# Splitting the row sums' reciprocals over 128 partitions by way of DRAM, one addition of exponentials moved to GpSimd, and the copies of an attention stage put in another order

## The chip, the cores and the metric

One core of one Trainium2 chip. The metric is the device time of one execution in microseconds. The core's engines, which run their own instruction streams and meet at semaphores: TensorE (PE), VectorE (DVE), ScalarE (ACT), GpSimd (POOL), and SyncE (SP), which here issues nearly all DMA transfers, in the order in which they are written.

## The reference

```python
# attention: batch 2, 8 heads, 768 tokens, head size 64
q_bits = (q @ proj > 0); k_bits = (k @ proj > 0)          # 6 sign bits each
mask = bucket(q_bits) == bucket(k_bits)                   # keys of the same bucket only
scores = where(mask, q @ k.T / 8, -1e9)
attn = exp(scores - max(scores)); attn /= (sum(attn) + 1e-9)
x = attn @ v                                              # to (1536 tokens, 512)
# layer 1
h = x @ w_in1 ; x = (maximum(h, 0) + alpha * minimum(h, 0)) @ w_out1      # 512 -> 2048 -> 512
# layer 2
h = x @ w_in2
P = a0 + a1*h + a2*h^2 + a3*h^3 ; Q = 1 + |b0|*|h| + |b1|*h^2
out = (P / (Q + 1e-6)) @ w_out2
```

All is float32. The kernel splits operands into a high part (fp32r) and the rest, and multiplies high by high, high by low and low by high.

## The kernel before, in words

**Attention** goes over 16 heads in 8 pairs; pair `j` holds heads `h = 2j + u`, u = 0 or 1, and u is also the slot of double-buffered tiles. Pairs 1 to 5 are one hardware loop (`over_pairs`), pairs 0, 6 and 7 are written out. `left` is 2 in all pairs but the last two (1, 0). A head has six chunks of 128 keys. For each chunk TensorE makes scores (keys on partitions, 768 queries in two halves; `scores_one` L534 and `scores_two` L539, two chunks ahead), ScalarE takes the exponential into `p[c]` (L696), and TensorE multiplies it with v (`values`, L560) into `ps_o`. Chunks go in groups of two (`begin` = 0, 2, 4); in a group come the scores, the first list of helper steps, in group 0 the two steps below, the values, then the second list.

Ahead of their head, for one or two heads later, run: **bits** (L475), sign bits of q and k, turned by VectorE (L984) into `bit01` and by GpSimd (`bit_rows`, L831) into the penalty rows `pen`; **a** (L479), the plain scores with penalty, of which VectorE takes row maxima from PSUM (L980, halves of 384; `s_a_free` counts them); and **m** (`turn`, L490/492), which transposes maxima and empty-row marks that GpSimd made (`row_stats`, `v_partial`). ScalarE copies these out (`stat_rows`, L743/745) and SP carries the stats into `q2` (`fill_stats`, L419); VectorE makes `v_sum` (L1004) from them.

In group 0, ahead of the values, stand `empty_rows` (L573), which starts the accumulation in `ps_o` for rows without a key, and `sums` of the head before (L584): 24 small matmuls with ones over `p_sum[0..2]`. VectorE makes each `p_sum[n] = p[2n] + p[2n+1]` (`add`, L1013), one behind each group. ScalarE copies the sums, 768 queries as 4 rows of 192 spread over 128 partitions in copies, to `den_row[u]` (L757); VectorE takes reciprocals of all 128x192 (L124), SP stores 4 rows to DRAM (`store_rows`, L112) and, once per pair, spreads them over 64 partitions each (`spread`, L120). GpSimd multiplies (`normalise`, L908), ScalarE and GpSimd split the result into `x_hi` and `x_lo`.

**The order is written out by hand** in each engine's `pair`. SP's, per head h: stats of head h+1, raw q and k of head h+4, v, the reciprocals' store of head h-1, then `fill_a` for head h+3 (high parts L355/356, penalty rows L360/361), `spread` (u = 0), and the eight copies into the operands of head h+2 (`fill_b_hi` L374 to L377, waits for the last values of head h; `fill_b_lo` L381 to L384). The high part itself is ScalarE's `split_qk` (L678), behind the exponential of step c = 4; it waits for the last copies that read this slot (`s_a_in`, `s_b_in`). GpSimd's `split_qk` (L822) makes the low part.

**The MLP layers** (from L1101) run over 3 tiles of 512 tokens and 16 chunks of 128 hidden columns. Weights of four chunks are split beforehand, the others during layer 1: SP loads them (`load`, L1206/1209), GpSimd splits (L1241 to L1252). The first two `up` chunks run inside the last pair.

Of the kernel before, what the change touches and what calls it, by code (L numbers as in the profile page):

```python
# [62 lines left out]
def build_program(nc, qk, v, proj, w_in1, w_out1, alpha, w_in2, w_out2, a, b, consts, out):  # L63
    rden_dram = nc.dram_tensor("rden_scratch", (PAIRS, 2, S), F32, kind="Internal").ap()
    outer = ExitStack()
    with outer:
# [23 lines left out]
        x32, rden_bc = work[:, 0:S], work[:, S:2 * S]  # L90
        guard = sb_in(outer, "guard", [P, 1])

        s_sums = sem("s_sums")
        s_rden = [sem(f"s_rden{u}") for u in range(2)]
        s_rst = [sem(f"s_rst{u}") for u in range(2)]
# [12 lines left out]
        def store_rows(sp, u, j, row):  # L108

            sp.wait_ge(s_rden[u], j + 1)  # L110
            dst = rden_dram[bass.ds(j, 1)].rearrange("a u (n t) -> (a u n) t", n=4)[4 * u:4 * u + 4]
            sp.dma_start(dst, row[0:P:QUARTER_ROWS]).then_inc(s_rst[u], 16)  # L112
# [19 lines left out]
        with att:  # L132
# [90 lines left out]
            s_add = sem("s_add")  # L223
            s_summed = sem("s_summed")
            s_pv = sem("s_pv")
            s_head = sem("s_head")
# [113 lines left out]
            def attention_sync(sp):  # L340
# [22 lines left out]
                def fill_a(u, jj):  # L363
                    g = 2 * jj + u
                    fill_a_hi(u, g)
                    fill_a_pen(u, g)

                def fill_b_hi(u, jj):
# [3 lines left out]
                    if due(g - 1):  # L372
                        sp.wait_ge(s_head, g - 1)
# [37 lines left out]
                def fill_stats(slot, jj):  # L411
# [3 lines left out]
                    if due(g - 1):  # L415
                        sp.wait_ge(s_head, g - 1)
# [17 lines left out]
                def pair(j, left):  # L434
                    for u in range(2):
                        h = 2 * j + u
                        if left == 1 and u == 0:
# [7 lines left out]
                        if isinstance(j, int) and j == 0:  # L445
# [15 lines left out]

            def attention_tensor(pe):
# [91 lines left out]
                def values(slot, h, c, t):  # L554

                    pe.wait_ge(s_exp, t + 1)
                    if c == 0:
                        pe.wait_ge(s_vhi, h + 1)
                    for i in range(2):
                        m = pe.matmul(ps_o[OUT[i], 0, 0:HALF], v_use[slot][:, c], p[c][:, i * HALF:(i + 1) * HALF],  # L560
                                      start=False, stop=(c == KC - 1))
                    m.then_inc(s_head if c == KC - 1 else s_pv, 1)

                def empty_rows(slot, h):

                    if isinstance(h, int) and h == 0:
                        pe.wait_ge(s_first_sum, 1)
                    else:
                        pe.wait_ge(s_a_free, turned(h))
                    if due(h):  # L570
                        pe.wait_ge(s_evac, h)
                    for i in range(2):
                        pe.matmul(ps_o[:, 0, 0:HALF], v_sum[slot][:, (1 - i) * D:(1 - i) * D + P],  # L573
# [1061 lines left out]
```

## Time and profile before

| | us |
|---|---|
| median of 3 runs | 853.35 |
| lowest, highest | 848.66, 853.62 |
| the profiled execution | 848.33 |
| its span in the profile | 846.3 |
| mean granted clock of TensorE | 0.969 of full |

| engine | busy us | share |
|---|---|---|
| TensorE, matmuls | 802.2 | 95% |
| VectorE | 558.6 | 66% |
| ScalarE | 358.3 | 42% |
| GpSimd | 269.7 | 32% |

Attention ends near 315 us, with the last sums' matmuls. An engine that waits shows as idle, and the profile names the engine or transfer that released it. The granted clock is a share of TensorE's full clock (2.4 GHz; the other level is 1.2). A share of busy time is a mean over stages with different limits, so the views by stretch of time say more than the totals.

### The profile page before, as it was taken

How to read it: one execution, taken by the hardware profiler on the slowest of the kernel's cores; microseconds unless marked ns; L12 is line 12 of the kernel's file. 1: busy time of each engine (PE TensorE's matmuls, PEld its weight loads, DVE VectorE, ACT ScalarE, POOL GpSimd, SP SyncE). 2: the span in 40 equal slices, each digit the busy share in tenths (PEclk: the TensorE clock that was granted, in tenths of full speed). 3: DMA queues.
4: the chain of work that ended last, by engine and by line, in shares of the span. 5: the costliest groups of instructions: out<-in, count | busy, mean ns of one | idle time of the engine just before them, and what ended most of it. 6: DMA issues, size and time to landing. Idle time of an engine off the chain costs nothing.

```text
span 846.3 us, 11668 instructions
## 1 busy us (share of the span) xinstructions
PE 802.2 (95%) x3820; PEld 589.4 (70%) x3820; DVE 558.6 (66%) x830; ACT 358.3 (42%) x588; POOL 269.7 (32%) x341
## 2 busy tenths in 40 slices
PE   8898888888888999999999999999999999999998
PEld 5455545454444667888888888888788888888886
DVE  6776676666666746544434344338988888888886
ACT  7343444434333541111201121116766676667664
POOL 7563443535355345970000017777000000000000
PEclk9999999988888999999999999999999999999999
DMA  4564464545444623420000003332000010001001
GB/s 127 146 179 130 111 156 110 129 112 135 119 131 119 149 72 117 119 81 1 0 1 1 13 0 100 92 95 75 1 2 1 0 50 2 0 1 50 2 1 50
DMA packets 29726, 58.75 MB, mean 69 GB/s; under 512 B 5420, under 2 KB 9300, under 8 KB 29684
## 3 DMA queue, kind: packets, MB, share of 16 engines
q1 hardware_dynamic: 29396, 58.16, 25.4%
q8 instruction: 25, 0.41, 0.2%
q14 instruction: 17, 0.14, 0.1%
q10 hardware_dynamic: 288, 0.04, 0.0%
HBM read 29.54 MB, written 3.19 MB: 39 GB/s over the span
## 4 chain that ended last, share of the span: by engine, by line
PE 82%; DVE 7%; DMA 4%; SPq 4%; issue 2%; ACT 0%; POOL 0%; DVEq 0%; ACTq 0%
PE acc L1311 29%; PE ps_h L1279 29%; PE ps_o L560 6%; PE ps_a L479 4%; DMA ka<-pen 3%; PE ps_s L534 3%; PE ps_s L539 3%; PE ps_o L584 3%; PE ps_a L475 2%; DVE den_row L124 2%; PE ps_o L573 1%; DVE row_max L980 1%; SPq L360 1%; SPq L112 1%; SPq L356 1%
## 5 line engine op out<-in xcount | busy, mean ns | idle before, releaser
L1344 ACT ACTIVATE g_hi<-num 128x512 fp32r<-128x512 f32 x96 | 59.9, 624 | 207.4 <-PE acc L1311 203.0
L1414 DVE TENSOR_TENSOR g_lo<-num,g_hi 128x512 fp32r<-128x512 f32 x96 | 70.7, 736 | 78.4 <-ACT g_hi L1344 77.9
L696 ACT ACTIVATE p<-ps_s 128x768 f32<-128x768 f32 x96 | 77.5, 810 | 98.1 <-PE ps_s L539 98.1
L980 DVE TENSOR_REDUCE row_max<-ps_a 128x1 f32<-128x384 f32 x180 | 90.9, 546 | 35.4 <-PE ps_a L479 33.6
L479 PE MATMUL ps_a<-ka,qa 76*128 76x384 f32 x180 | 63.3, 408 | 33.4 <-DMA ka<-pen 31.4
L1013 DVE TENSOR_TENSOR p_sum<-p 128x768 f32<-128x768 f32 x48 | 68.6, 1431 | 27.7 <-PE ps_o L584 27.2
L479 PEld LDWEIGHTS ps_a<-ka,qa 76*128 76x128 f32 x180 | 31.9, 196 | 68.9 <-issue 36.4
L1279 PE MATMUL ps_h<-x_hi,w_late_in_hi 128*128 128x512 f32 x288 | 78.9, 395 | 1.0 <-POOL w_late_in_lo L1243 1.0
L1279 PE MATMUL ps_h<-x_hi,w_late_in_lo 128*128 128x512 f32 x288 | 77.7, 392 | 0.0
L1279 PE MATMUL ps_h<-x_lo,w_late_in_hi 128*128 128x512 f32 x288 | 77.6, 391 | 0.0
L560 PE MATMUL ps_o<-p,v_use 128*64 128x384 f32 x384 | 73.7, 502 | 0.0
L1422 DVE TENSOR_SCALAR num<-ps_h,alpha_sb 128x512 f32<-128x512 f32 x48 | 36.0, 750 | 55.9 <-PE ps_h L1279 53.3
L1352 ACT ACTIVATE den_q<-ps_h,abs_b 128x512 f32<-128x512 f32 x48 | 33.1, 690 | 82.7 <-PE ps_h L1279 76.5
L1279 PEld LDWEIGHTS ps_h<-x_hi,w_late_in_hi 128*128 128x128 f32 x288 | 54.0, 188 | 13.8 <-POOL w_late_in_lo L1243 1.4
L1279 PEld LDWEIGHTS ps_h<-x_lo,w_late_in_hi 128*128 128x128 f32 x288 | 54.1, 188 | 12.1
L1279 PEld LDWEIGHTS ps_h<-x_hi,w_late_in_lo 128*128 128x128 f32 x288 | 54.1, 188 | 12.0
L1311 PE MATMUL acc<-w_late_out_hi,g_hi 128*128 128x512 f32 x144 | 56.8, 395 | 0.0
L1311 PE MATMUL acc<-g_hi,w_late_out_hi 128*128 128x512 f32 x144 | 56.6, 393 | 0.0
L1311 PE MATMUL acc<-w_late_out_lo,g_hi 128*128 128x512 f32 x144 | 56.5, 392 | 0.0
L1311 PE MATMUL acc<-g_hi,w_late_out_lo 128*128 128x512 f32 x144 | 56.5, 392 | 0.0
L1311 PE MATMUL acc<-g_lo,w_late_out_hi 128*128 128x512 f32 x144 | 56.2, 390 | 0.0
L1311 PE MATMUL acc<-w_late_out_hi,g_lo 128*128 128x512 f32 x144 | 56.1, 390 | 0.0
(167 smaller groups left out, 1584.0 us busy)
## 6 DMA issues: line engine op xcount, KB each, us to landing
stage<-in_w_in SPq DMA_DIRECT2D x26, 256.0 KB, 2.8
stage<-in_w_out SPq DMA_DIRECT2D x26, 256.0 KB, 2.8
raw<-in_qk SPq DMA_DIRECT2D x15, 384.0 KB, 3.2
q<-hi SPq DMA_DIRECT2D x30, 192.0 KB
k<-hi SPq DMA_DIRECT2D x30, 192.0 KB
v_raw<-in_v SPq DMA_DIRECT2D x16, 192.0 KB, 3.0
work<-rden_scratch SPq DMA_DIRECT2D x16, 192.0 KB, 3.4
out<-y SPq DMA_DIRECT2D x12, 256.0 KB, 2.5
```

Source lines behind the costliest of these rows:

```text
L479: m = pe.matmul(ps_a[:, i, 0:HALF], qa[slot][0:BIT_ROW + 12, c * P:(c + 1) * P], ka[slot][0:BIT_ROW + 12, half], start=True, stop=True)
L534: pe.matmul(ps_s[c % 2][:, i, 0:HALF], k1[slot][:, c * P:(c + 1) * P], q1[slot][:, i * HALF:(i + 1) * HALF], start=True, stop=False)
L560: m = pe.matmul(ps_o[OUT[i], 0, 0:HALF], v_use[slot][:, c], p[c][:, i * HALF:(i + 1) * HALF], start=False, stop=(c == KC - 1))
L696: nc.scalar.activation(halves(p[c][:]), ps_s[c % 2][:, :, 0:HALF], ACT.Exp, scale=float(D) ** -0.5).then_inc(s_exp, 1)
L980: dve.tensor_reduce(row_max[slot][:, i, c:c + 1], ps_a[:, i, 0:HALF], AX.X, ALU.max).then_inc(s_a_free, 1)
L1013: dve.tensor_tensor(p_sum[n][:], p[2 * n][:], p[2 * n + 1][:], ALU.add).then_inc(s_add, 1)
L1279: m = pe.matmul(ps_h[f % 4][:], weight(w, f)[:, k * P:(k + 1) * P], tile_cols(x, t, k), start=(n == 0), stop=(n == 3 * DK - 1))
L1311: m = pe.matmul(acc[d][:], lhs, rhs, start=(f == 0 and n == 0), stop=(f == FC - 1 and n == 2))
L1344: nc.scalar.activation(g_hi[f % 2][:], num[f % 4][:], ACT.Copy).then_inc(s_ghi, 1)
L1352: nc.scalar.activation(den_q[f % 2][:], h, ACT.Abs, scale=abs_b[:, 0:1])
L1414: dve.tensor_tensor(g_lo[f % 2][:], num[f % 4][:], g_hi[f % 2][:], ALU.subtract).then_inc(s_glo, 1)
L1422: dve.tensor_scalar(num[f % 4][:], h, 0.0, alpha_sb[:, f:f + 1], ALU.min, ALU.mult).then_inc(s_step, 1)
```

## The change

The order of heads, chunks and helper steps on TensorE stays; `empty_rows` goes from ahead of the values to behind those of chunk 3, so the values of chunk 0 start the accumulation. `p_sum[1]` (chunks 2 and 3) is made by GpSimd. The copied sums go to DRAM as they are; per pair, they are read back as 6 values per partition and slot, VectorE takes the reciprocals of 128x12 values once, behind the last group of the even head, and they go to DRAM again ahead of `spread`. ScalarE's `split_qk` goes from step 4 to step 1. SP's order is new, and the b copies wait for `empty_rows` and no longer for the last values.

```diff
+        def store_sums(sp, u, j, h, row):
+            sp.wait_ge(s_sums, h + 1)
+            dst = den_dram[bass.ds(j, 1)].rearrange("a u (n t) -> (a u n) t", n=4)[4 * u:4 * u + 4]
+            sp.dma_start(dst, row[0:P:QUARTER_ROWS]).then_inc(s_dst[u], 16)
+        def turn_sums(sp, j):
+            for u in range(2):
+                sp.wait_ge(s_dst[u], 16 * (j + 1))
+            if due(j):
+                sp.wait_ge(s_rden, j)
+            for u in (1, 0):
+                src = den_dram[bass.ds(j, 1)].rearrange("a u s -> (a u) s")[u:u + 1].rearrange("a (p c) -> (a p) c", c=KC)
+                sp.dma_start(den[:, u], src).then_inc(s_den, 16)
+        def store_rows(sp, j):
+            sp.wait_ge(s_rden, j + 1)
+            dst = rden_dram[bass.ds(j, 1)].rearrange("a u (p c) -> p (a u) c", c=KC)
+            sp.dma_start(dst, rden[:]).then_inc(s_rst, 16)
         def spread(sp, j):
+            sp.wait_ge(s_rst, 16 * (j + 1))
             for u in range(2):
-                sp.wait_ge(s_rst[u], 16 * (j + 1))
-            for u in (1, 0):
...
-        def reciprocal(dve, u, h, row):
-            dve.wait_ge(s_sums, h + 1)
-            dve.reciprocal(row, row).then_inc(s_rden[u], 1)
+        def reciprocals(dve, j):
+            dve.wait_ge(s_den, 32 * (j + 1))
+            if due(j):
+                dve.wait_ge(s_rst, 16 * j)
+            dve.reciprocal(rden[:], den[:]).then_inc(s_rden, 1)
...  SP, fill_b_hi and fill_stats
-                        sp.wait_ge(s_head, g - 1)
+                        sp.wait_ge(s_rows, g - 1)
...  SP, pair(j, left), for u in range(2)
-                        if left or u == 0:
-                            fill_stats(1 - u, j + u)
                         if left > 1:
                             load_raw(u, j + 2)
                         if left:
                             load_v(u, j + 1)
...
-                        if not (isinstance(h, int) and h == 0):
-                            store_rows(sp, 1 - u, j - 1 + u, den_row[1 - u][:])
+                        if first and u == 0:
+                            fill_stats(1 - u, j + u)
                         if left > 1 or (left == 1 and u == 0):
-                            fill_a(1 - u, j + 1 + u)
-                        if u == 0 and not (isinstance(j, int) and j == 0):
-                            spread(sp, j - 1)
+                            fill_a_hi(1 - u, h + 3)
+                        if not (first and u == 0):
+                            store_sums(sp, 1 - u, j - 1 + u, h - 1, den_row[1 - u][:])
+                        if (left or u == 0) and not (first and u == 0):
+                            fill_stats(1 - u, j + u)
+                        if left > 1 or (left == 1 and u == 0):
+                            fill_a_pen(1 - u, h + 3)
+                        if u == 0 and not first:
+                            turn_sums(sp, j - 1)
                         if left:
                             fill_b_hi(u, j + 1)
+                        if u == 0 and not first:
+                            store_rows(sp, j - 1)
                         if left:
                             fill_b_lo(u, j + 1)
+                        if u == 0 and not first:
+                            spread(sp, j - 1)
...  TensorE, values(slot, h, c, t), c == 0
+                        if due(h):
+                            pe.wait_ge(s_evac, h)
...
-                                      start=False, stop=(c == KC - 1))
-                    m.then_inc(s_head if c == KC - 1 else s_pv, 1)
+                                      start=(c == 0), stop=(c == KC - 1))
+                    m.then_inc(s_pv, 1)
...  TensorE, sums(h)
-                    pe.wait_ge(s_add, KC // 2 * (h + 1))
+                    pe.wait_ge(s_add, 2 * (h + 1))
+                    pe.wait_ge(s_add_too, h + 1)
...  TensorE, pair
-                            if begin == 0:
-                                empty_rows(u, h)
-                                if not first:
-                                    sums(h - 1)
+                            if begin == 0 and not first:
+                                sums(h - 1)
                             for c in range(begin, begin + group):
                                 values(u, h, c, KC * h + c)
+                                if c == 3:
+                                    empty_rows(u, h)
...  ScalarE, exponential(c, h, t)
-                        act.wait_ge(s_add, KC // 2 * (h - 1) + c // 2 + 1)
...
+                        if c // 2 == 1:
+                            act.wait_ge(s_add_too, h)
                         else:
-                            act.wait_ge(s_pv, (KC - 1) * (h - 1) + c + 1)
+                            act.wait_ge(s_add, 2 * (h - 1) + c // 4 + 1)
+                        act.wait_ge(s_pv, KC * (h - 1) + c + 1)
...  ScalarE, pair
+                            if c == (4 if first and u == 0 else 1) and (left > 1 or (left == 1 and u == 0)):
+                                split_qk(1 - u, j + 1 + u)
                             if c == 3 and not last:
                                 copy_v(1 - u, j + u)
-                            if c == 4 and (left > 1 or (left == 1 and u == 0)):
-                                split_qk(1 - u, j + 1 + u)
-                            if c == (2 if final else 3) and u == 1 and not first:
+                            if c == (2 if final else 5) and u == 1 and not first:
                                 x_high(act, j - 1)
...  GpSimd
+                def add(n, h):
+                    pool.wait_ge(s_exp, KC * h + 2 * n + 2)
+                    if due(h):
+                        pool.wait_ge(s_summed, h)
+                    nc.gpsimd.tensor_tensor(p_sum[n][:], p[2 * n][:], p[2 * n + 1][:], ALU.add).then_inc(s_add_too, 1)
...  GpSimd, pair: normalise from ahead of bit_rows to behind split_qk
                         if left > 1 or (left == 1 and u == 0):
                             bit_rows(1 - u, j + 1 + u)
+                        add(1, h)
+                        if left > 1 or (left == 1 and u == 0):
+                            split_qk(1 - u, j + 1 + u)
...  VectorE, pair
-                                if side == 0 and (begin + group) % 2 == 0:
+                                if side == 0 and begin + group in (2, KC):
                                     add((begin + group) // 2 - 1, h)
-                            if begin == 2 and not (first and u == 0):
-                                reciprocal(dve, 1 - u, h - 1, den_row[1 - u][:])
+                            if begin == 4 and u == 0 and not first:
+                                reciprocals(dve, j - 1)
...  handover to the MLP, SP
-                store_rows(sp, 1, PAIRS - 1, rden_bc[:, 0:QUARTER])
+                store_sums(sp, 1, PAIRS - 1, HEADS - 1, rden_bc[:, 0:QUARTER])
+                turn_sums(sp, PAIRS - 1)
+                store_rows(sp, PAIRS - 1)
                 spread(sp, PAIRS - 1)
```

## Rows read from the trace of the kernel before

**Rows 1.** The page, TensorE's granted clock in 40 equal slices, tenths of full.
```profile
PEclk9999999988888999999999999999999999999999
```
**Rows 2.** Stretches: busy time (instructions) per engine, granted clock, DMA share, GB/s.
```profile
160.00:200.00 40.00, 34.38 (x184) 19.95 (x182) 26.11 (x40) 15.65 (x26) 16.57 (x26) 0.83 0.49 124
...
280.00:320.00 40.00, 39.98 (x255) 26.08 (x255) 24.48 (x34) 20.97 (x36) 17.17 (x24) 1.00 0.39 101
```
**Rows 3.** TensorE's waits, whole span: total us, times, longest.
```profile
PE ps_a L479 <- DMA ka<-pen: 31.4, 12, 2.9
...
PE ps_h L1279 <- POOL w_late_in_lo L1243: 1.0, 1, 1.0
```
**Rows 4.** The chain of waits, 165 to 174 us: start, us, what.
```profile
166.41 1.27 DVE den_row L124
...
167.83 0.61 SPq L112
...
170.65 2.29 DMA ka<-pen
```
**Rows 5.** TensorE's timeline, marks of several heads: start, us, engine, line, operation.
```profile
39.73 0.52 PE L534 MATMUL ps_s<-q,k 128*128 128x384 f32 x2
...
41.91 0.84 PE L475 MATMUL ps_a<-raw,pj 128*24 128x384 f32 x4
42.69 0.62 PE L573 MATMUL ps_o<-q,v_sum 128*128 128x384 f32 x2
...
47.05 0.51 PE L479 MATMUL ps_a<-ka,qa 76*128 76x384 f32 x2
...
156.29 1.01 PE L573 MATMUL ps_o<-q,v_sum 128*128 128x384 f32 x2
...
169.44 0.52 PE L534 MATMUL ps_s<-q,k 128*128 128x384 f32 x2
...
173.06 1.00 PE L479 MATMUL ps_a<-ka,qa 76*128 76x384 f32 x2 [2.74 <-DMA ka<-pen]
...
258.49 1.01 PE L573 MATMUL ps_o<-q,v_sum 128*128 128x384 f32 x2
...
276.77 0.51 PE L573 MATMUL ps_o<-q,v_sum 128*128 128x384 f32 x2
...
290.23 0.51 PE L573 MATMUL ps_o<-q,v_sum 128*128 128x384 f32 x2
```
**Rows 6.** The stretch behind the wait of head 8, columns as rows 2.
```profile
174.00:179.30 5.30, 5.30 (x35) 2.45 (x33) 2.02 (x4) 0.81 (x1) 0.00 (x0) 0.53 0.76 182
```
**Rows 7.** VectorE, ScalarE, GpSimd near head 8; first, L1013's min/median/max in ns.
```profile
L1013 DVE TENSOR_TENSOR p_sum<-p x48: 894/964/2396, 24.4 to 311.5; 128x768 f32<-128x768 f32 x48
...
161.45 0.29 DVE L1004 SCALAR_TENSOR_TENSOR v_sum<-vs_hi,cst,ps_a 4x64 fp32r<-4x64 f32 x1 [1.32 <-ACT vs_hi L745]
...
167.16 0.84 ACT L678 ACTIVATE hi<-raw 128x768 fp32r<-128x768 f32 x1
...
168.08 1.83 POOL L822 TENSOR_TENSOR lo<-raw,hi 128x768 fp32r<-128x768 f32 x1 [1.12 <-ACT hi L678]
...
168.46 2.26 DVE L1013 TENSOR_TENSOR p_sum<-p 128x768 f32<-128x768 f32 x1
...
171.68 0.17 DVE L994 TENSOR_REDUCE top<-row_max 128x6 f32<-128x12 f32 x1
```
**Rows 8.** DMA issues: queue, count, KB each, median us to landing.
```profile
ab_raw<-in_b SPq DMA_DIRECT2D x1, 1.0 KB, 3.3
```
**Rows 9.** SP's issues in head 8, first and last of the four b-lo copies.
```profile
174.02 0.73 SPq L381 DMA_DIRECT2D k<-lo  x1
...
176.74 0.77 SPq L384 DMA_DIRECT2D k<-pen  x1
```
**Rows 10.** The handover to the MLP: VectorE's last reciprocal, SP's next load of weights.
```profile
323.15 1.35 DVE L124 RECIPROCAL work<-work 128x192 f32<-128x192 f32 x1
...
327.45 0.57 SPq L1206 DMA_DIRECT2D stage<-in_w_in  x1
```

More of the change, by code:

```diff
@@ L90, in build_program @@
         x32, rden_bc = work[:, 0:S], work[:, S:2 * S]
+        den = sb_in(outer, "den", [P, 2, KC])
+        rden = sb_in(outer, "rden", [P, 2, KC])
         guard = sb_in(outer, "guard", [P, 1])
         s_sums = sem("s_sums")
-        s_rden = [sem(f"s_rden{u}") for u in range(2)]
-        s_rst = [sem(f"s_rst{u}") for u in range(2)]
+        s_dst = [sem(f"s_dst{u}") for u in range(2)]
+        s_den = sem("s_den")
+        s_rden = sem("s_rden")
+        s_rst = sem("s_rst")
         s_rbc = sem("s_rbc")
@@ L223, in build_program @@
             s_add = sem("s_add")
+            s_add_too = sem("s_add_too")
             s_summed = sem("s_summed")
             s_pv = sem("s_pv")
-            s_head = sem("s_head")
+            s_rows = sem("s_rows")
             s_evac = sem("s_evac")
@@ L436, in pair @@
                         h = 2 * j + u
+                        first = isinstance(j, int) and j == 0
                         if left == 1 and u == 0:
                             stage_early(2)
-                        if left or u == 0:
-                            fill_stats(1 - u, j + u)
                         if left > 1:
@@ L444, in pair @@
                             load_v(u, j + 1)
-                        if isinstance(j, int) and j == 0:
+                        if first:
                             stage_early(u)
@@ L558, in values @@
                         pe.wait_ge(s_vhi, h + 1)
+                        if isinstance(h, int) and h == 0:
+                            pe.wait_ge(s_first_sum, 1)
+                        if due(h):
+                            pe.wait_ge(s_evac, h)
                     for i in range(2):
                         m = pe.matmul(ps_o[OUT[i], 0, 0:HALF], v_use[slot][:, c], p[c][:, i * HALF:(i + 1) * HALF],
-                                      start=False, stop=(c == KC - 1))
-                    m.then_inc(s_head if c == KC - 1 else s_pv, 1)
+                                      start=(c == 0), stop=(c == KC - 1))
+                    m.then_inc(s_pv, 1)
                 def empty_rows(slot, h):
-                    if isinstance(h, int) and h == 0:
-                        pe.wait_ge(s_first_sum, 1)
-                    else:
+                    if not (isinstance(h, int) and h == 0):
                         pe.wait_ge(s_a_free, turned(h))
-                    if due(h):
-                        pe.wait_ge(s_evac, h)
                     for i in range(2):
-                        pe.matmul(ps_o[:, 0, 0:HALF], v_sum[slot][:, (1 - i) * D:(1 - i) * D + P],
-                                  q2[slot][:, i * HALF:(i + 1) * HALF], start=(i == 0), stop=False)
+                        m = pe.matmul(ps_o[:, 0, 0:HALF], v_sum[slot][:, (1 - i) * D:(1 - i) * D + P],
+                                      q2[slot][:, i * HALF:(i + 1) * HALF], start=False, stop=False)
+                    m.then_inc(s_rows, 1)
                 def sums(h):
-                    pe.wait_ge(s_add, KC // 2 * (h + 1))
+                    pe.wait_ge(s_add, 2 * (h + 1))
+                    pe.wait_ge(s_add_too, h + 1)
                     if due(h):
@@ L940, in pair @@
                             row_stats(1 - u, h + 1)
-                        if u == 1 and not final and not (isinstance(j, int) and j == 0):
-                            normalise(j - 1)
                         if left > 1 or (left == 1 and u == 0):
                             bit_rows(1 - u, j + 1 + u)
+                        add(1, h)
+                        if left > 1 or (left == 1 and u == 0):
+                            split_qk(1 - u, j + 1 + u)
                         if left == 1 and u == 0:
@@ L947, in pair @@
                         if u == 1 and not final and not (isinstance(j, int) and j == 0):
+                            normalise(j - 1)
                             x_low(j - 1)
-                        if left > 1 or (left == 1 and u == 0):
-                            split_qk(1 - u, j + 1 + u)
                         if isinstance(j, int) and j == 0:
@@ L1529, in mlp_vector @@
                 step(0, 0, 0, False, None)
-                reciprocal(dve, 1, HEADS - 1, rden_bc[:, 0:QUARTER])
+                reciprocals(dve, PAIRS - 1)
                 def tile(layer, t, final):
```

23 lines of the change are left out of this document (7 added, 16 removed).

## The prediction

> **What bounds the kernel now.** The page comes first: TensorE's clock row sags in slices 9 to 14 and is full afterwards [rows 1]; a reader is to see a stage there that the rest of the span doesn't resemble. The view by stretches says where there is something to gain: from 160 to 200 us TensorE is busy 34.38 of 40 us at a mean clock of 0.83, from 280 to 320 us 39.98 of 40 at 1.00 [rows 2]. The two MLP layers behind are TensorE work without gaps, and the change doesn't touch them. So only attention, some 315 of 846 us, can move. Third, the waits of TensorE: 31.4 us in 12 waits, all for the same transfer, the penalty rows of `ka` [rows 3]. One per head, in heads 2 to 13.
>
> Fourth, the chain of waits through one of them, in head 8 [rows 4]. VectorE's reciprocal (1.27) ends, SP stores its rows (0.61), and behind that, in SP's order, stand the four copies into `qa` and `ka`; the last lands 2.29 us after its issue, and TensorE starts again at 173.06 after 2.74 us [rows 4, 5]. The wait costs twice: from 174.0 to 179.3 the granted clock is 0.53, near 1.2 of 2.4 GHz [rows 6]. In the timeline the empty-rows matmul, one pair per head, marks the heads: 42.69 in head 1, 276.77 in head 13, so 234.1 us for twelve heads, 19.5 each. From head 13 to head 14 TensorE doesn't wait: 13.46 us [rows 5].
>
> **What a head costs without the wait.** The head 13 stretch lacks two pieces, the bits matmuls (0.84, of which 0.8 in sequence) and one row-maximum pair (0.51 with its overlap, 0.4 in sequence) [rows 5]: 13.46 + 1.2 = 14.7; 14.8 with a little for VectorE's order. Twelve heads make 177.6.
>
> **The change, part by part.** *The penalty transfer.* ScalarE's split of q and k goes from behind chunk 4 to behind chunk 1; SP fills `qa`/`ka` before the sums' store, and no reciprocal stands in the way. I count from T, the start of the scores of chunk 2 (169.44 in head 8) [rows 5]. ScalarE copies the sums near T+4.2 (42.69 - 39.73 = T+3.0 in head 1, where the sums' matmuls begin, and some 1.2 us of them), splits by T+5.1, and SP issues two hi copies, the store (0.6), the stats, two penalty copies: done by T+9.4, landed (2.3) by T+11.7. It is wanted after T+15. All twelve old waits go: that is the 31.4 us and the low clock behind them.
>
> *The reciprocals.* Per head 1.34 us on 192 elements goes, for one of 12 elements per pair; the nearest row for a tiny operation is 0.17 [rows 7]. The pair's sums make a round trip: store, two loads of 24-byte pieces, reciprocal, store in 24-byte pieces, spread. No such transfer is in the trace; the nearest moves 1.0 KB in small pieces, 8 bytes to a partition, and lands in 3.3 us; the two steps of the store seen here are an issue of 0.61 and a landing near the 2.29 of the penalty rows [rows 4, 8]. I take 2.5, the nearer to the size, with both ends kept, and SP issues of 0.6. Loads are issued by T+10.9 in the even head and landed by T+13.4; VectorE asks for them only behind the last maximum of that head, 2.2 us into the next. Four microseconds of cover; past that it costs one for one.
>
> The Trainium skill (DMA: Bandwidth & Descriptors, "Why small descriptors are slow") holds small pieces to and from HBM to be slow, and speaks against this layout. The one small row at 3.3 us against 2.29 is no proof either way; by that rule the cover would shrink, and the sum would not change before it is used up.
>
> *What it leaves late.* SP's order in the even head is: turn, b-hi copies, wait for the reciprocals, store, b-lo copies. The reciprocals come 2.2 us into the odd head (its top reduction stands at 171.68, T+2.2, with a reciprocal less ahead of it) [rows 7]. Store to T+2.9; the four b-lo copies take 3.5 (174.02 to 177.51), to T+6.4 [rows 9]; landing 2.3, to T+8.7. ScalarE's split, now at chunk 1, waits for exactly these copies, and it arrives at T+4.2. Behind it in ScalarE's queue stand the stats copy and the partial-sum copy, and VectorE's `v_sum` behind them: 0.84 and 0.29 [rows 7], and some 0.3 at most for each small copy between, an estimate, to T+10.1. TensorE gets to the second half of the next row-maximum pair at 47.05 - 39.73 = 7.3 in head 1, 6.8 without the empty rows that move back [rows 5]. So it waits 3.3 us, in every odd head that has this split: 1, 3, 5, 7, 9, 11 (head 1 because SP is late from the weights). Six waits for twelve. The clock's fall after a wait cost from nothing to 2.9 us: from head 7 (156.29) to head 12 (258.49) a head takes 20.4 us, and 20.4 - 14.8 - 2.74 = 2.9; from head 1 to head 7 18.9, which leaves 1.4, and the reciprocals may account for it all [rows 5]. I take 1.5, since a pair has one wait where it had two. Odd heads: +4.8, six times, 28.8.
>
> *The even heads.* Copies to the odd head's operands end near T+21.7 of a 19.6 us head, landed at about T+2.1 of the next: no wait there. SP's own queue per pair is some 23 us of issues and 2 more, in 34.
>
> *The addition on GpSimd.* VectorE loses one of three additions (0.96 alone); GpSimd gains one that costs what its own of this shape costs, 1.83 [rows 7]. GpSimd is busy 16.57 of 40 us in 160 to 200 [rows 2], some 8.5 per head, and would be at 10.3 in 17. Its end matters to the sums matmuls and two exponentials of the next head, five us later. Cost nothing, the cover being those five us.
>
> *Empty rows behind chunk 3, the waits on counts:* same work, no cost; the b copies may start earlier, but SP isn't free earlier.
>
> *The handover to the MLP.* Before, the last store waits for a reciprocal that VectorE reaches at 323.15, and the late weights are issued at 327.45 [rows 10]. Now the store goes at about 318, loads landed by 323.3, reciprocal at 323.4, store, landing, spread, weights at 327.2. A wash; the 1.0 us wait of TensorE stays [rows 3].
>
> **The sum.** 177.6 + 28.8 = 206.4 for 234.1: minus 27.7 on the profiled execution of 848.3 (span 846.3), so 820.6. That execution is like the lowest of the three runs (848.66); their median is 5 us higher, where the same difference gives 825.7. I forecast 822. Bounds from the open terms: no odd waits at all, 791.8; odd waits with the full clock loss (37.2) and 1.3 us per head from colliding additions (15.6), 844.6.
>
> **The rivals.**
> *A, odd waits hidden.* If b-lo copies are ready by T+6, the wait shrinks to about 1 us and the clock stays: 177.6 + 6 to 12, or 798 to 811. For: early heads lost little clock. Against: SP's order is written out. 0.15.
>
> *B, the additions collide.* In the trace VectorE's addition from 168.46 takes 2.26 and ends 0.8 behind GpSimd's subtraction of 168.08 to 169.91; over all 48 the median is 0.964, the longest 2.396 [rows 7]. With 1.83 us more of GpSimd per head, and every addition of VectorE a gate for ScalarE's buffers and the reductions behind it, it can lose 1.3 per head: 15.6 more, 836, and with the clock up to 845. Against: one exposed addition fewer, and VectorE is busy 26.11 of 40 [rows 2]. 0.20. The Trainium skill (SBUF: State Buffer, "SBUF: two separate sides") makes it a rule: an addition with both inputs in SBUF and a GpSimd operation exclude each other for a whole instruction. The overlapped row agrees.
>
> *C, slower: the turned sums don't arrive.* VectorE's queue holds the reciprocals before the next head's reductions. If the loads landed over 6.7 us after issue, VectorE, and with it TensorE, would stand, once a pair in six pairs. It decides from where it eats 27.7 + 8.5: 6 us per pair, a landing of about 13 us. At 15 us: 820.6 + 6 x 8 = 869. For: no row has 24-byte pieces, and the store has 256 of them. Against: 3.3 us is the longest near row. 0.08.
>
> *D, no change.* The head isn't shortened, since TensorE gives the same time to waits for row maxima and low clock: 846 to 856. Against: head 13. 0.05.
>
> **How the numbers follow.** The forecast's case, 811 to 832, has 0.52. The range, 803 to 842, leaves out part of A, the end of B, C and D: two in ten. One per cent, what a measurement of this kernel can tell from no change, is 8.5 us. Faster: 0.52 + 0.15 + over half of B = 0.79. Slower: C, 0.08. Within: 0.13.
>
> **What would show it.** The waits for `ka<-pen` gone from TensorE; waits on `v_sum` or ScalarE's stats at T+7 in odd heads only, about 3 us each; ScalarE's split waiting for `q<-pen`/`k<-pen` there; empty rows of heads 1 and 13 206 us apart; reciprocals with no wait on a transfer; VectorE's additions not much over 1.2 us in the mean. I am wrong if even heads wait too, if the odd wait is absent, or if the low clock outlasts the odd head.

## The result, and the profile after

| | before | after |
|---|---|---|
| median, us (4 runs each) | 851.00 | 807.96 |
| lowest, highest | 837.89, 853.62 | 805.44, 808.44 |
| span of the profiled execution | 846.3 | 805.8 |
| mean granted clock of TensorE | 0.969 | 0.996 |

After over before is 0.9575, with a 95% interval of 0.9466 to 0.9685: 4.2% faster, 14 us below the forecast of 822 and inside the range. Executions of the kernel before spread over 837.7 to 857.2 us on the chips used here, with mean granted clocks from 0.987 to 0.953; the ratios leave out those far above its fastest one, where the two medians alone would give 5.1%. Versions close to each other are therefore compared with each other.

The page of the kernel after, engine totals and the clock in 40 slices:

```profile
PE 784.4 (97%) x3820; PEld 587.1 (73%) x3820; DVE 513.3 (64%) x806; ACT 360.0 (45%) x588; POOL 295.8 (37%) x357
...
PEclk9899999999999999999999999999999999999999
```

The sag of the clock in slices 9 to 14 [rows 1] is gone. By stretch (columns as [rows 2]), the one that stood at 34.38 busy us and a clock of 0.83:

```profile
160.00:200.00 40.00, 37.32 (x225) 23.19 (x224) 24.59 (x46) 20.06 (x32) 23.63 (x33) 1.00 0.60 147
```

TensorE runs 225 matmul instructions there where it ran 184. Its waits (total us, times, longest):

```profile
PE ps_s L566 <- DMA q<-stats: 7.7, 7, 2.3
PE ps_a L506 <- DVE v_sum L1040: 4.2, 6, 0.8
...
PE ps_h L1317 <- POOL w_late_in_lo L1281: 0.3, 1, 0.3
```

All twelve waits for `ka<-pen`, 31.4 us [rows 3], are gone. Six waits on `v_sum` are new. Of the seven on the stats rows of `q2`, a transfer that the forecast had not in mind, one (2.3 us, in head 0) has its like in the kernel before (1.9 us); the other six, 5.5 us, stand in the odd heads 1 to 11. The empty-rows matmuls again mark the heads, 1 to 13 (start, us, what); they now stand behind chunk 3. The scores of chunk 2, called T in the prediction, are the same place in both kernels, so those of heads 1 and 13 are shown too:

```profile
41.94 0.51 PE L561 MATMUL ps_s<-q,k 128*128 128x384 f32 x2
...
52.55 0.62 PE L600 MATMUL ps_o<-q,v_sum 128*128 128x384 f32 x2
...
232.00 0.52 PE L561 MATMUL ps_s<-q,k 128*128 128x384 f32 x2
...
241.26 0.62 PE L600 MATMUL ps_o<-q,v_sum 128*128 128x384 f32 x2
```

The kernel before, head 13:

```profile
272.28 0.52 PE L534 MATMUL ps_s<-q,k 128*128 128x384 f32 x2
```

188.7 us for twelve heads, where it was 234.1 [rows 5] and 206.4 was forecast. Between these two marks lie five of the waits on `v_sum` (3.6 us; head 1's comes earlier) and six of those on the stats (5.5 us). Without them a head takes 179.6 / 12 = 14.97 us.

The marks give 45.4 us less, but the whole span is only 40.5 us shorter. The marks do not stand at the same distance from T in heads 1 and 13 (T+3.0 and T+4.5 before, T+10.6 and T+9.3 after), which makes 2.9 us of the difference, and head 1 begins 2.2 us later than before (41.94 for 39.73 [rows 5]). From T to T the twelve heads take 190.1 us where they took 232.6.

One odd head, 5, whose scores of chunk 2 begin at T = 104.90. First the timeline of the engines, then SP's issues:

```profile
104.90 0.52 PE L561 MATMUL ps_s<-q,k 128*128 128x384 f32 x2
...
106.10 0.23 DVE L146 RECIPROCAL rden<-den 128x12 f32<-128x12 f32 x1
...
111.14 0.84 ACT L707 ACTIVATE hi<-raw 128x768 fp32r<-128x768 f32 x1 [1.50 <-DMA k<-pen]
...
112.42 0.29 DVE L1040 SCALAR_TENSOR_TENSOR v_sum<-vs_hi,cst,ps_a 4x64 fp32r<-4x64 f32 x1 [2.23 <-ACT vs_hi L774]
...
112.76 0.44 PE L506 MATMUL ps_a<-ka,qa 76*128 76x384 f32 x1 [0.71 <-DVE v_sum L1040]
...
117.24 0.62 PE L566 MATMUL ps_s<-q,k 128*128 128x384 f32 x2 [0.25 <-DMA q<-stats]
```

```profile
103.13 0.61 SPq L395 DMA_DIRECT2D k<-hi  x1
106.35 0.42 SPq L133 DMA_DIRECT2D rden_scratch<-rden  x1
106.82 0.48 SPq L399 DMA_DIRECT2D k<-lo  x1
...
108.82 0.76 SPq L402 DMA_DIRECT2D k<-pen  x1
...
113.75 0.61 SPq L117 DMA_DIRECT2D den_scratch<-den_row  x1
114.46 0.72 SPq L437 DMA_DIRECT2D q<-stats  x1
```

The forecast chain is here link by link. SP has its b-hi copies out at 103.74, stands until the tiny reciprocal at 106.10, stores it, issues the four b-lo copies (106.82 to 109.58), the last lands near 111.1, and ScalarE's split, `v_sum` and TensorE's next row-maximum matmul follow. Only the lengths differ. The last rows show one thing more: the stats stand behind all of that and behind the store of the sums, and TensorE meets them too.

VectorE's additions (min/median/max in ns), and the new small transfers (count, KB, median us to landing):

```profile
L1049 DVE TENSOR_TENSOR p_sum<-p x32: 957/959/2069, 24.1 to 269.1; 128x768 f32<-128x768 f32 x32
```

```profile
den<-den_scratch SPq DMA_DIRECT2D x16, 3.0 KB, 1.6
...
rden_scratch<-rden SPq DMA_DIRECT2D x8, 6.0 KB, 2.1
```

### The profile page after: what moved, and what is told of

The parts are those of the page before. It is cut to its first block, busy times and chain, and to the rows that moved or that the text cites. A ratio compares the mean times of both kernels' runs of the same rounds, so it can differ in the third digit from the quotient of the medians.

```text
span 805.8 us, 11708 instructions
## 1 busy us (share of the span) xinstructions
PE 784.4 (97%) x3820; PEld 587.1 (73%) x3820; DVE 513.3 (64%) x806; ACT 360.0 (45%) x588; POOL 295.8 (37%) x357
## 4 chain that ended last, share of the span: by engine, by line
PE 82%; SPq 6%; DVE 4%; DMA 4%; issue 2%; POOL 1%; ACT 1%; DVEq 0%; ACTq 0%; POOLq 0%
PE acc L1349 31%; PE ps_h L1317 30%; PE ps_o L591 6%; PE ps_a L506 4%; PE ps_s L566 3%; DMA q<-stats 3%; PE ps_s L561 3%; PE ps_o L613 1%; PE ps_a L502 1%; SPq L140 1%; DVE row_max L1016 1%; PE ps_o L600 1%; SPq L401 1%; SPq L117 1%; PE ps_s L620 1%
## 5 line engine op out<-in xcount | busy, mean ns | idle before, releaser
L1382 ACT ACTIVATE g_hi<-num 128x512 fp32r<-128x512 f32 x96 | 59.9, 624 | 206.4 <-PE acc L1349 202.1
L506 PE MATMUL ps_a<-ka,qa 76*128 76x384 f32 x180 | 60.0, 384 | 5.5 <-DVE v_sum L1040 4.2
L566 PE MATMUL ps_s<-q,k 128*128 128x384 f32 x192 | 50.9, 346 | 8.6 <-DMA q<-stats 7.7
```

What stands on the lines that cost most here:

```text
L506: m = pe.matmul(ps_a[:, i, 0:HALF], qa[slot][0:BIT_ROW + 12, c * P:(c + 1) * P], ka[slot][0:BIT_ROW + 12, half], start=True, stop=True)
L566: m = pe.matmul(ps_s[c % 2][:, i, 0:HALF], k2[slot][:, c * P:(c + 1) * P], q2[slot][:, i * HALF:(i + 1) * HALF], start=False, stop=True)
L1382: nc.scalar.activation(g_hi[f % 2][:], num[f % 4][:], ACT.Copy).then_inc(s_ghi, 1)
```

## The experiments

Times are medians; "ratio" is to the kernel before on the same chip, with a 95% interval. Four kernels (the addition alone, the early split alone, the addition back, the reciprocals back) have no ratio; the kernel before stood at 854.10 us beside them (838.06 to 856.68). The recorded expectations call the chunks of `p_sum[1]` 3 and 4; counted from 0, as here, they are 2 and 3.

### The parts on the kernel before

**The addition alone.** `p_sum[1]` made by GpSimd, nothing else.

```diff
+                def add(n, h):
+                    ...
+                    nc.gpsimd.tensor_tensor(p_sum[n][:], p[2 * n][:], p[2 * n + 1][:], ALU.add)
...  VectorE
-                                if side == 0 and (begin + group) % 2 == 0:
+                                if side == 0 and begin + group in (2, KC):
```

> The kernel before with the addition of chunks 3 and 4 on GpSimd alone. My theory: VectorE isn't on the path there, the reciprocal starts at the same time behind the same row maximum, so within 1%, the waits for ka<-pen stay at 12 and about 31 us. The rival (VectorE's relief): 12 heads by about 1 us, ratio 0.985 or less.

851.14 us (848.83 to 852.73). TensorE's wait on `ka<-pen` stays, 33.4 us in 12, as expected. No gain is shown.

**The early split and the penalty copies alone.** ScalarE's `split_qk` behind chunk 1, SP's `fill_a` ahead of `store_rows`.

```diff
+                        if left > 1 or (left == 1 and u == 0):
+                            fill_a(1 - u, j + 1 + u)
                         if not (isinstance(h, int) and h == 0):
                             store_rows(sp, 1 - u, j - 1 + u, den_row[1 - u][:])
...  ScalarE
-                            if c == 4 and (left > 1 or (left == 1 and u == 0)):
+                            if c == (4 if first and u == 0 else 1) and (left > 1 or (left == 1 and u == 0)):
                                 split_qk(1 - u, j + 1 + u)
```

> The kernel before with one part of the change: ScalarE's split at step 1, and SP's four copies into qa and ka ahead of the reciprocals' store; reciprocals, additions and all else as before. My theory, that the gain comes from taking the reciprocal and its store out of the way of the penalty rows: the 31.4 us of waits for ka<-pen go, but the split now waits for the b copies in every head (they still wait for the last values), so a wait of about 2 us on v_sum takes their place; some 17.8 us per head in place of 19.5, 20 us less, ratio 0.97 to 0.98. The rival, that VectorE's relief brings the gain: no change, within 1%.

840.56 us (836.95 to 843.52). TensorE's waits:

```profile
PE ps_a L479 <- DVE v_sum L1004: 31.2, 12, 4.5
```

ScalarE's, in attention:

```profile
ACT hi L678 <- DMA k<-pen: 40.8, 12, 5.3
```

The wait for `ka<-pen` is gone and one of the same size has its place, in every head: the split now comes before the b copies that free its slot. This version stands 13.5 us under the median of the kernel before on this chip, and not under its shortest execution, 838.06, so a gain is not shown; 20 us were expected. Even by the median, taking the named wait away is worth under a third of the whole change.

**The empty rows alone.** Empty rows behind chunk 3, the b copies released by them.

```diff
-                            if begin == 0:
-                                empty_rows(u, h)
-                                if not first:
-                                    sums(h - 1)
+                            if begin == 0 and not first:
+                                sums(h - 1)
                             for c in range(begin, begin + group):
                                 values(u, h, c, KC * h + c)
+                                if c == 3:
+                                    empty_rows(u, h)
...  SP, fill_b_hi
-                        sp.wait_ge(s_head, g - 1)
+                        sp.wait_ge(s_rows, g - 1)
```

> The kernel before with one part of the change: the empty rows' matmuls behind chunk 3's values, b copies and stats waiting for them and no longer for the last values. The split stays at step 4 and the reciprocals' store ahead of the qa/ka copies. My theory: alone it brings nothing, since SP reaches the b copies later than the last values anyway, 845 to 856 and 12 waits for ka<-pen. The rival, that the early release is the main part by itself: 835 or less.

853.51 us (853.19 to 855.28). The kernel before took 837.73 to 857.20 beside it, median 851.82; the ratio is 1.0157 (1.0127 to 1.0186). Neither shows a gain, as expected; the waits for `ka<-pen` are the same 31.4 us in 12.

**Both together.** The last two edits in one kernel, in short:

```diff
-                                empty_rows(u, h)
...  TensorE, behind values(u, h, c, KC * h + c)
+                                if c == 3:
+                                    empty_rows(u, h)
...  SP
+                            fill_a(1 - u, j + 1 + u)
                         if not (isinstance(h, int) and h == 0):
                             store_rows(sp, 1 - u, j - 1 + u, den_row[1 - u][:])
```

> Both parts together on the kernel before: empty rows behind chunk 3, and split at step 1 with the qa/ka copies ahead of the store. Reciprocals of 128x192, all additions on VectorE. My theory, that these two need each other and are the whole gain: neither alone moves more than 2%, together 797 to 805. The rival, that relief of VectorE by the turned reciprocals or GpSimd's addition is needed as well: 808 or more.

844.21 us (10 executions, 838.81 to 848.14), ratio 1.0036 (0.9994 to 1.0078). A clear miss: I held these two for the whole gain. TensorE's waits, and SP's issues in one even head, whose T is 113.67:

```profile
PE ps_a L479 <- DVE v_sum L1002: 34.1, 11, 5.3
```

```profile
109.97 0.76 SPq L361 DMA_DIRECT2D ka<-pen  x1
112.11 0.60 SPq L112 DMA_DIRECT2D rden_scratch<-den_row  x1
113.91 1.27 SPq L120 DMA_DIRECT2D work<-rden_scratch  x2
115.36 0.52 SPq L374 DMA_DIRECT2D q<-hi  x1
...
120.71 0.77 SPq L384 DMA_DIRECT2D k<-pen  x1
```

The empty rows had released the b copies at 109, and SP didn't send them before 115.36: it stood for VectorE's reciprocal, stored, stood for the landing, spread. They end at T+7.8 and the split starts at T+10.6, with 5.96 us of waiting. The release was there and SP's order made nothing of it. SP's waits in attention, from 40 to 290 us, say the same for all heads:

```profile
SPq L419 <- ACT stats L741: 36.9, 12, 3.8
SPq L112 <- DVE den_row L124: 35.7, 13, 5.3
```

It stands for the stats and for the reciprocals, and besides them only for the store's landing (6.0 us in 6), never for the empty rows.

### The parts of the kernel after

**The addition back on VectorE.**

```diff
-                        add(1, h)
...  VectorE
-                                if side == 0 and begin + group in (2, KC):
+                                if side == 0 and (begin + group) % 2 == 0:
```

> The changed kernel with that addition back on VectorE, all else as changed. My theory: VectorE has room now, at most 0.3 us per head, 808 to 812. The rival: gives back 12 us or more, 820 and above.

809.26 us (808.57 to 810.44), against 807.96 for the kernel after, as expected. The two were measured apart, so 1.3 us is no difference to build on: no worth of GpSimd's addition is shown.

**The reciprocals of 128x192 back on VectorE,** without the turn through DRAM; SP's store of a head's rows stands between b-hi and b-lo copies.

```diff
-                        if u == 0 and not first:
-                            turn_sums(sp, j - 1)
                         if left:
                             fill_b_hi(u, j + 1)
-                        if u == 0 and not first:
-                            store_rows(sp, j - 1)
+                        if not (first and u == 0):
+                            store_rows(sp, 1 - u, j - 1 + u, den_row[1 - u][:])
...  VectorE
-                            if begin == 4 and u == 0 and not first:
-                                reciprocals(dve, j - 1)
+                            if begin == 2 and not (first and u == 0):
+                                reciprocal(dve, 1 - u, h - 1, den_row[1 - u][:])
```

> The changed kernel with the reciprocals of 128x192 on VectorE in each head again and no turning through DRAM; their store stands behind the b-hi copies, where the changed kernel stores the turned ones. My theory: nothing hangs on the reciprocals any more there, and the b-lo copies no longer wait for the end of the even head, so the odd heads' waits on v_sum go too: 800 to 810, as fast as the changed kernel. The rival (VectorE's relief is what pays): 12 to 15 heads by 1.3 us more, 823 or above.

798.64 us (797.85 to 799.50), 9.3 less than the kernel after, and 10.6 less than the 809.26 on the same chip, where the addition differs too. TensorE's waits:

```profile
PE ps_s L540 <- DMA q<-stats: 2.4, 2, 2.2
...
PE ps_a L480 <- DVE v_sum L1014: 1.0, 1, 1.0
```

The part that gives the change its name costs time. VectorE again spends 1.34 us per head on reciprocals, and TensorE loses nothing by it: the chain of b-lo copies through a mid-pair reciprocal is gone, and so are nearly all waits for stats.

**Both back,** the last two edits in one kernel, in short, so that VectorE does all that it did before and only the order of work is new.

```diff
-                                reciprocals(dve, j - 1)
...
+                                reciprocal(dve, 1 - u, h - 1, den_row[1 - u][:])
...
-                        add(1, h)
```

> a_wide (798.6) with the addition of chunks 3 and 4 back on VectorE, which then does all that it did before. My theory: there VectorE is near its limit, some 13 of 15 us per head, and each delay of a row maximum is seen: 0 to 0.4 us per head, 799 to 804. The rival, that GpSimd's addition costs more by collisions than it frees: faster than 798.

798.64 us (797.68 to 800.23), ratio 0.9494 (0.9468 to 0.9520): the fastest version, with the one above, which has the addition on GpSimd and the same time; the expectation (799 to 804) and its rival (under 798) both miss it narrowly. Against "both together" it differs in SP's order, in GpSimd's (its split ahead, `normalise` behind it) and in ScalarE's (`x_high` at step 5 for 3). SP, in an even head with T = 104.48:

```profile
100.30 0.53 SPq L369 DMA_DIRECT2D q<-hi  x1
...
102.98 0.62 SPq L112 DMA_DIRECT2D rden_scratch<-den_row  x1
103.65 0.82 SPq L376 DMA_DIRECT2D k<-lo  x1
...
105.99 0.77 SPq L379 DMA_DIRECT2D k<-pen  x1
107.01 1.28 SPq L120 DMA_DIRECT2D work<-rden_scratch  x2
```

The b copies leave as the empty rows release them (a matmul at 99.60), end at T+2.3 where they ended at T+7.8, and the split starts at 108.98 without a wait. SP's largest wait in attention is now for the empty rows:

```profile
SPq L368 <- PE ps_o L573: 20.9, 13, 3.6
```

**The empty rows one chunk later,** in the kernel with the wide reciprocals (behind chunk 4 for 3).

```diff
-                                if c == 3:
+                                if c == 4:
                                     empty_rows(u, h)
```

> The changed kernel with the reciprocals of 128x192 back on VectorE (a_wide, 798.6) and the empty rows' matmuls behind the values of chunk 4 in place of chunk 3, so that SP's b copies are released about 3 us later. My theory now, that their early release by the empty rows is a main part of the gain, since the split of the next head but one waits for them: a wait on v_sum of about 1.5 us in nearly every head, 812 to 822. The rival, that SP isn't free earlier anyway (as the prediction said): no change, 798 to 800.

834.86 us (833.13 to 836.48), ratio 0.9825 (0.9750 to 0.9901): 36 more than without the edit, and more than expected. TensorE's waits:

```profile
PE ps_a L480 <- DVE v_sum L1014: 16.0, 11, 2.4
PE ps_s L540 <- DMA q<-stats: 9.4, 8, 2.6
```

With SP's order right, the release is the gate: SP waits 59.8 us for these matmuls from 40 to 270 us, and each of the heads 2 to 12 takes 16.5 us or more from T to T, where they took 14.8 to 15.2.

**More stores behind the reciprocals.** The kernel after, with 3 or 7 further stores of `rden` (to DRAM that nobody reads) ahead of the b-lo copies in the even heads 2 to 12, so that the odd wait grows. The spread waits for these stores too; the order of work is the same.

```diff
+            if more:
+                for n in range(3):
+                    ...
+                    sp.dma_start(to, rden[:].rearrange("p a c -> p (a c)")).then_inc(s_rst, 16)
```

> The changed kernel with three more stores of the 128x12 reciprocals to unread DRAM ahead of the b-lo copies of each even head (six times), so that the copies come about 1.3 us later. This sets the wait that I had forecast too long. By the step of the prediction: the odd wait grows from 0.7 to some 2 us, six times 1.3 us, 816; with a fall of the clock behind each wait up to 2.9 us more, 825 to 833.

> As a_late3 with seven more stores, about 3 us: the odd wait about 3.8 us, which spans the 3.3 us that the prediction priced. If the clock holds, 6 x 3.1 us: 826. If it falls as in the kernel before (2.9 us per wait in its late heads), 840 to 845 and a clock below 0.98; the prediction's middle value of 1.5 gives 835.

822.00 us (821.88 to 822.56), ratio 0.9667 (0.9594 to 0.9740), and 839.43 us (838.16 to 840.09), ratio 0.9868 (0.9792 to 0.9943). TensorE's waits with 3, then with 7:

```profile
PE ps_a L516 <- DVE v_sum L1050: 12.1, 6, 2.3
PE ps_s L576 <- DMA q<-stats: 6.0, 4, 2.3
```

```profile
PE ps_a L516 <- DVE v_sum L1050: 23.8, 6, 5.5
PE ps_s L576 <- DMA q<-stats: 6.4, 3, 3.2
```

Both times lie between what was expected without a fall of the clock and with its largest. Against 4.2 and 7.7, three stores add 7.9 - 1.7 = 6.2 us to these two waits and 14.0 us to the time; seven add 19.6 - 1.3 = 18.3 and 31.5. So TensorE loses more than the waits. What it loses besides them isn't the same each time, though. Head 1's wait stayed at 0.6 us, and those of the odd heads 3 to 11 grew to 2.3 us with three stores. Here, with three stores, are the stretch behind the wait that ends at 82.91, and the wait that ends at 219.75 with the stretch behind it; then a wait of the kernel after with its stretch (columns as [rows 2], the granted clock third from the end):

```profile
83.00:89.00 6.00, 6.00 (x18) 3.58 (x19) 2.02 (x4) 1.59 (x3) 5.12 (x3) 0.52 0.66 179
...
219.75 0.44 PE L516 MATMUL ps_a<-ka,qa 76*128 76x384 f32 x1 [2.30 <-DVE v_sum L1050]
...
220.00:225.00 5.00, 3.99 (x21) 2.43 (x20) 2.84 (x6) 1.44 (x3) 4.99 (x3) 1.00 0.80 208
```

```profile
181.80 0.62 PE L566 MATMUL ps_s<-q,k 128*128 128x384 f32 x2 [1.88 <-DMA q<-stats]
...
182.00:188.00 6.00, 5.98 (x31) 3.92 (x31) 4.19 (x8) 4.46 (x7) 2.58 (x3) 1.00 0.77 185
```

The same wait of 2.3 us is followed by a clock of 0.52 once and of 1.00 another time. An odd head of the kernel after takes 14.9 us from T to T without its waits; taking that and the waits off, the odd heads 3 to 11 lose 2.7, 1.7, 1.6, 1.5 and 0.0 us more with three stores (1.5 in the mean), and 1.7, 2.4, 2.7, 2.9 and 3.0 us with seven, behind waits of 5.5 and 4.4 (2.5 in the mean). The forecast took 1.5 us behind 3.3. So a further loss behind the wait is shown, of the size forecast or somewhat more, with a spread as large as itself. At the forecast's 3.3 us these two versions give, by a straight line through the totals, 833, an estimate.

**The b-lo copies ahead of the reciprocals' store.** The kernel after.

```diff
-                        if u == 0 and not first:
-                            store_rows(sp, j - 1)
                         if left:
                             fill_b_lo(u, j + 1)
+                        if u == 0 and not first:
+                            store_rows(sp, j - 1)
```

> The changed kernel with one step of SP moved: in the even head the four b-lo copies go ahead of the wait for the turned reciprocals, their store behind. My theory, that the odd heads' waits come from these copies standing behind the reciprocals: the six waits on v_sum (4.2 us) go, and the stats, which stand behind the copies in SP's queue there, arrive earlier, so most of the 7.7 us for q<-stats goes too: 797 to 801, as a_wide. The rival, that the sums' way through DRAM costs by its small transfers whatever their place: 805 or more.

Six executions: 804.94, 804.65, and four of 811.08 to 811.32; ratio 0.9541 (0.9469 to 0.9614). TensorE's waits in one of the shorter ones:

```profile
PE ps_s L566 <- DMA q<-stats: 7.8, 6, 2.3
...
PE ps_a L506 <- DVE v_sum L1040: 0.5, 1, 0.5
```

The waits on `v_sum` are gone but for one, as theory had it, but the 797 to 801 us that it gave did not come. SP now stands for the landing of the store ahead of the spread, 13.0 us in 8, and the stats behind it come no earlier. Why this version has two times, 6.4 us apart, stays open: the trace is of a shorter one, and the mean clocks, 0.996 and 0.998 against 0.989 to 0.995, are close. Whether the three more transfers per pair cost by themselves, the rival, stays open with it.

**And the spread moved** into the next odd head, behind its penalty copies; the last edit stays.

```diff
                             fill_a_pen(1 - u, h + 3)
+                        if u == 1 and left and not (isinstance(j, int) and j == 0):
+                            spread(sp, j - 1)
```

> The changed kernel with the b-lo copies ahead of the reciprocals' store (a_blo_first, whose waits for q<-stats stayed) and the spread moved into the odd head, behind its penalty copies, so that SP never stands for the landing of the turned reciprocals. My theory, that SP's queue and not the transfers' landing makes what is left: the stats waits of odd heads go to under 2 us in total, 797 to 802. The rival, that three more transfers per pair cost by themselves: stays at 804 to 811.

817.98 us (814.63 to 818.88), ratio 0.9731 (0.9704 to 0.9758). TensorE's waits:

```profile
PE ps_a L519 <- POOL mcols L918: 12.4, 6, 2.5
PE ps_s L568 <- DMA q<-stats: 2.9, 2, 2.3
```

GpSimd's:

```profile
POOL work L946 <- DMA work<-rden_scratch: 35.6, 7, 8.9
```

The stats came early, as expected. But GpSimd's `normalise` stands for the late spread, and behind it in GpSimd's order stand the marks (`mcols`) that TensorE transposes. Another miss: with the turn through DRAM each place in SP's order that I tried made someone wait.

## Why the prediction was right, and where it wasn't

The time was in the range, but not in the case that the forecast held likeliest (811 to 832): 807.96 lies in the interval that rival A was given. The odd waits with their clock came out 25.2 us smaller than forecast, and other terms 7.5 us larger; that these partly cancel was luck.

**What bounds the kernel:** right. Only attention moved, by the waits for `ka<-pen` and the low clock behind them.

**A head without waits, 14.8:** 14.97 measured, 2.0 us over twelve heads.

**The penalty transfer:** all twelve waits went. What I didn't say is that this alone is worth little: the release by the empty rows and a new place for the b copies in SP's order had to be there as well.

**The reciprocals:** no wait of VectorE for their loads shows among its waits. The loads, issued from 100.22, land 1.6 us later; VectorE reaches them at T+1.2 (I said T+2.2). The pieces of 24 bytes cost 1.6 and 2.1 us where I took 2.5, below both ends that I kept. Rival C needed 13. The 1.0 KB transfer that I went by landed in 3.3 us in the kernel before and in 4.7 us in the kernel after, so one such row carries little. The Trainium skill (DMA: Bandwidth & Descriptors, "Why small descriptors are slow") spoke against this layout; the landings of 1.6 and 2.1 us for 3 and 6 KB show nothing of it.

**What it leaves late:** the mechanism and its six heads (1, 3, 5, 7, 9, 11) were right, and this is the term that was mis-sized. I built T+8.7 for the split from 2.2 for VectorE, 0.7 for the store, 3.5 for four copies and 2.3 for the landing. Measured: 1.2, 0.7, 2.8 and 1.5, so T+6.2. The first row was long because it held an addition of 2.26 us where most took 0.96 [rows 7]; why the copies were issued faster here isn't shown (four of them at 88.32 in the same trace took 3.4). A wait is what is left when the need is taken off, and TensorE came to its need at T+7.1 where I had T+6.8: so 0.7 was left of 3.3. In this trace the clock did not fall behind it, so that the 1.5 went as well: 4.2 us in place of 28.8. The store experiments show that a loss behind longer waits is there, of 0 to 2.7 us behind 2.3.

**The clock in the early heads:** I read from rows 5 that heads 1 to 7 may have lost nothing by it. That was wrong. In the kernel before the granted clock is 0.57 from 97 to 101 us, behind the 2.75 us of head 4, and it falls behind the waits of heads 3, 6 and 7 too; it is 1.00 from 115.4 to 120 us, behind the 2.84 us of head 5.

**The even heads:** no waits on `v_sum`, right.

**Not foreseen:** the stats, 5.5 us in six waits of odd heads, behind the store of the sums and the hi copies in SP's order. This gave a part back. The working between the marks closes: 206.4 forecast, less 25.2 for the waits on `v_sum` and their clock (28.8 less 3.6), 2.0 more for the heads without waits, and 5.5 more for the stats, is the 188.7 measured. Of the 17.7 us less than forecast the execution shows 12.9 (807.7 for 820.6): nearly all of the rest is the marks' places and the later start of head 1.

**The addition on GpSimd at nothing:** right, by an edit each way, and once more by 798.64 us with it and without it. VectorE's additions have a mean of 1.09 us, so rival B's 1.3 per head isn't there. The Trainium skill (SBUF: State Buffer, "SBUF: two separate sides") has an addition of VectorE with both inputs in SBUF and a GpSimd operation that reads SBUF exclude each other for a whole instruction; single additions did take up to 2.07 us, but the median is 0.96.

**Empty rows: "same work, no cost; ... SP isn't free earlier":** wrong. With the wide reciprocals, one chunk later costs 36 us. I read SP's freedom from the order of the kernel before, where the store and the spread do hold it, and the change takes them away.

**The handover a wash:** right; its wait is 0.3 us, was 1.0.

**Rival A** is what came: odd waits near 1 us and a full clock. I had given it 0.15 since the chain is written out; the chain's place was right, its sum was not. A's own sum, 6 to 12 us of waits, gives 798 to 804 and not 798 to 811; that 807.96 is above it is due to the stats and the longer heads.

What isn't shown: how much of the difference between "both together" and the fastest version is GpSimd's order or the later `x_high`, since they were never parted from SP's order. SP's waits speak for its own order, but no edit changed that alone.

## What to carry to other kernels

A wait that the profile names is often the first of several in a row: here neither early copies, nor an early release, nor both were worth much until the queue that issues them stopped standing for something else ahead of them. When a step moves, follow the issuing queue with its new order and not with its old one. And a predicted wait is a small difference of long sums: quote it as a range that reaches down to zero, and price the clock's fall behind it as a range as well.

## What was unexpected in the hardware

What a wait of TensorE costs besides itself can't be told from its length alone. The granted clock stayed at 1.00 behind 0.7 us and once behind 1.88; behind five waits of 2.3 us the further loss was 0.0 to 2.7 us, and behind five of 4.4 to 5.5 us it was 1.7 to 3.0, the least behind the longest (these losses are estimates from the lengths of the heads). And 24-byte pieces, 128 to 256 of them, landed in 1.6 and 2.1 us, with 0.42 us for SP to issue the store, less than the 0.6 of the large copies.
